# Clustered attention and two MLPs: the second batch's cluster lots spread over the first pair's steps, their loads one by one behind the moves

## The reference

```
q_assign = argmax(q_n . c_n)          k_assign = argmax(k_n . c_n)
mask   = q_assign[..., :, None] == k_assign[..., None, :]
scores = where(mask, scale * q @ k.T, -1e9)
attn   = softmax(scores);  x = attn @ v
x -> x @ w_in (512x2048), h * sigmoid(1.702 h), @ w_out (2048x512)
x -> x @ w_in2 (512x1024), SoLU, layer norm * g_ln, @ w_out2 (1024x512)
```

## Time and profile before

| | |
|---|---|
| median of 3 runs | 667.44 us |
| the profiled execution | 669.38 us, its span 667.5 us (1.88 us around it) |
| PE busy | 640.2 us, 96% of the span |
| DVE, ACT, POOL busy | 465.6, 354.6, 443.1 us |
| granted clock of PE, mean | 0.987 |
| chain that ended last | PE 74%, ACT 10%, issue 6%, DVE 5%, DMA 3% |

### The profile page before, as it was taken

One profiled execution on the slowest core, in us unless ns is written; L12 is line 12 of the kernel. 1 busy time (PEld: TensorE's weight loads), 2 busy tenths in 40 slices (PEclk: granted clock), 3 DMA queues, 4 the chain that ended last, 5 costly groups with the idle time before them and its releaser, 6 DMA issues.

```text
span 667.5 us, 11328 instructions
## 1 busy us (share of the span) xinstructions
PE 640.2 (96%) x3311; PEld 539.5 (81%) x3311; DVE 465.6 (70%) x796; ACT 354.6 (53%) x709; POOL 443.1 (66%) x584
## 2 busy tenths in 40 slices
PE   7779999999999999999999999999999999999998
PEld 4449899898989898888878888878888888888876
DVE  3259999999999996564644684855457478778660
ACT  3149999999999985333325344443332144443241
POOL 3137787987988877766675777676666776867100
PEclk9788999999999999999999999999999999999999
DMA  8946645445545340222222222222220000000001
GB/s 253 281 129 166 148 108 155 123 108 149 135 108 143 91 172 32 95 92 93 99 95 95 90 92 100 96 94 88 100 96 32 0 1 16 33 11 22 32 31 48
DMA packets 26937, 64.32 MB, mean 96 GB/s; under 512 B 3872, under 2 KB 10016, under 8 KB 26912
## 3 DMA queue, kind: packets, MB, share of 16 engines
q1 hardware_dynamic: 25184, 60.87, 31.2%
q10 hardware_dynamic: 1728, 3.15, 1.3%
HBM read 46.51 MB, written 4.72 MB: 77 GB/s over the span
## 4 chain that ended last, share of the span: by engine, by line
PE 74%; ACT 10%; issue 6%; DVE 5%; DMA 3%; DVEq 1%; SPq 1%; POOL 0%; ACTq 0%
PE banks L610 7%; PE banks L640 7%; PE banks L625 7%; PE banks L642 7%; PE banks L627 7%; PE banks L626 7%; PE banks L641 7%; PE banks L595 4%; ACT probs L866 4%; PE banks L770 3%; PE banks L741 3%; PE banks L772 3%; PE banks L739 3%; PE banks L771 3%; PE banks L740 3%
## 5 line engine op out<-in xcount | busy, mean ns | idle before, releaser
L1112 DVE TENSOR_TENSOR probs_tl<-banks,probs_th 128x384 fp32r<-128x384 f32 x192 | 100.6, 547 | 11.8 <-ACT probs_th L877 8.4
L1408 POOL TENSOR_TENSOR wait_scrap<-half_power 128x1 f32<-128x1 f32 x128 | 26.1, 204 | 124.6 <-PE banks L642 67.0
L1092 DVE TENSOR_REDUCE neg_max<-banks 128x1 f32<-128x768 f32 x96 | 91.2, 950 | 7.5 <-PE banks L582 5.5
L877 ACT CAST probs_th<-banks 128x384 fp32r<-128x384 f32 x192 | 83.2, 486 | 21.9 <-PE banks L595 20.4
L866 ACT ACTIVATE probs<-banks,neg_max 128x768 f32<-128x768 f32 x96 | 88.2, 919 | 6.1 <-DVE neg_max L1092 6.0
L1484 POOL TENSOR_SCALAR probs<-probs,row_inv 128x768 f32<-128x768 f32 x96 | 87.0, 907 | 0.0
L1086 DVE TENSOR_TENSOR gl<-gate,gh 128x512 fp32r<-128x512 f32 x48 | 40.3, 839 | 63.5 <-ACT gh L851 63.5
L595 PE MATMUL banks<-ident,probs 128*128 128x128 f32 x576 | 80.1, 275 | 0.7 <-DVE hot_t L1064 0.7
L610 PE MATMUL banks<-probs_th,v_parts 128*128 128x384 f32 x192 | 70.4, 367 | 8.9 <-DVE x_sums L1119 8.9
L1467 POOL TENSOR_TENSOR downl<-gelu_raw,downh 128x512 fp32r<-128x512 f32 x48 | 75.8, 1580 | 4.0
L640 PE MATMUL banks<-gh,downh 128*128 128x512 f32 x192 | 76.0, 396 | 0.4 <-POOL downl L1467 0.2
(11 more groups left out here) (152 smaller groups left out, 1437.6 us busy)
## 6 DMA issues: line engine op xcount, KB each, us to landing
gelu_raw<-w_gelu SPq DMA_DIRECT2D x48, 512.0 KB, 3.3
ln_raw<-w_ln SPq DMA_DIRECT2D x8, 512.0 KB, 4.6
pair_t<-q_t SPq DMA_DIRECT2D x4, 768.0 KB, 7.2
kq_raw<-k_t SPq DMA_DIRECT2D x16, 192.0 KB, 3.5
kq_raw<-q_t SPq DMA_DIRECT2D x16, 192.0 KB, 3.6
pair_t<-k_t SPq DMA_DIRECT2D x4, 768.0 KB, 9.7
q_parts<-k_high SPq DMA_DIRECT2D x16, 192.0 KB, 2.6
q_high<-k_high SPq DMA_DIRECT2D x16, 192.0 KB, 3.0
```

The lines of the kernel that those rows point to most:

```text
L1092: nc.vector.tensor_reduce(out=neg_max[:, col], in_=scores[n % 2], op=ALU.max, axis=mybir.AxisListType.XY, negate=True).then_inc(max_done, 1)
L1112: nc.vector.tensor_tensor(probs_tl[half % 2][at], pt_bank(n, c).rearrange("p (t s) -> p t s", t=CH), probs_th[half % 2][at].bitcast(F32), ...
```

## The change

- Lots 4 to 7 all pass through pair 0's steps, one stage a step: lot e has its sims in step e - 3, its tokens in e - 2, ties in e - 1, first in e. Lot 7's ties are in step 6 and its first in step 7.
- Their sims go to PSUM bank 4, their tokens to bank 5, their ties and first to banks 6 and 7 as before; with this come other waits: sims of lot e > 4 wait until lot e - 1's sims have been copied, tokens of lot e for `compare(e - 1)`.
- The first `turn` (step 6) waits for `compared` = 8 alone, that of step 7 for `ties_t_copied` = 8, and `hot_t_done` = 8 is waited for in step 9.
- `keep_warm` ahead of the first scores is 20 turns in one piece.
- On SP the third move of head 0's k stands ahead of head 1's k and q; the load of lot 5 stands behind head 0's cluster rows, that of lot 6 behind head 1's third move, that of lot 7 behind head 1's last cluster rows, v and gains behind that.

```diff
-        def sims_t_ps(e):
-            return sims[e % 2] if e >= LATE_LOT else banks[:, e % 4, 0:HALF]
+            return banks[:, 4 if e >= 4 else e, 0:HALF]
+        def sims_ps(e):
+            return sims[1 if e >= 4 else e % 2]
-        SIMS_STEP = {6: 1, 7: 3}
...
+        SIMS_STEP = {e: e - 3 for e in range(4, LOTS)}
+        TOKENS_STEP = {e: e - 2 for e in range(4, LOTS)}
+        TIES_STEP = {e: e - 1 for e in range(4, LOTS)}
+        FIRST_STEP = {e: e for e in range(4, LOTS)}
                 move(q_parts[j][high, :], k_low[j][high, :], low_moved[j])
-                if isinstance(it, int) and it == 0 and j == 0:
+                sp.wait_ge(high_moved[j], (it + 1) * 32)
+                move(k_high[j][high, :], k_high[j][low, :], qk_ready[j])
+                if first and j == 0:
                     load_kq(0, 1)
                     load_pairs(4)
-                sp.wait_ge(high_moved[j], (it + 1) * 32)
-                move(k_high[j][high, :], k_high[j][low, :], qk_ready[j])
-                if isinstance(it, int) and it == 0 and j == 0:
-                    load_pairs(5)
+                if first and j == 1:
+                    cluster_rows(q_high[j][D:AUG, :], 0)
+                    load_pairs(6)
                 sp.wait_ge(low_moved[j], (it + 1) * 16)
-                for x, rows in enumerate((q_high[j], k_low[j])):
-                    cluster_rows(rows[D:AUG, :], x)
+                if not (first and j == 1):
+                    cluster_rows(q_high[j][D:AUG, :], 0)
+                cluster_rows(k_low[j][D:AUG, :], 1)
...
             place_head(0, 0)
-            for e in range(6, LOTS):
-                load_pairs(e)
-            sp.dma_start(gains_sb[:], gains).then_inc(gains_loaded, 16)
+            load_pairs(5)
+            place_head(0, 1)
+            load_pairs(7)
             for j in range(2):
                 load_v(0, j)
-            place_head(0, 1)
+            sp.dma_start(gains_sb[:], gains).then_inc(gains_loaded, 16)
...
             first_of(3)
-            sims_of(4)
-            keep_warm(6)
-            tokens_of(4)
-            sims_of(5)
-            ties_of(4)
-            tokens_of(5)
-            first_of(4)
-            keep_warm(16)
+            keep_warm(20)
...
                     if first and n == TURN_LAG + AHEAD:
+                        pe.wait_ge(compared, LOTS)
+                    if first and n == TURN_LAG + AHEAD + 1:
+                        pe.wait_ge(ties_t_copied, LOTS)
+                    if first and n == HEAD_LAG + AHEAD + CH - 1:
                         pe.wait_ge(hot_t_done, LOTS)
```

On ACT, in `attention_turn`:

```diff
+                    if isinstance(it, int) and it == 0 and TURN_LAG < n == TIES_STEP[LOTS - 1]:
+                        copy_ties(LOTS - 1)
                     if exists(it, n, TURN_LAG, STEPS) and not (drain and n >= TURN_LAG):
                         turned_high(*lagged(it, n, TURN_LAG, STEPS))
```

More of the change, by code:

```diff
@@ L88, in clustered_attention_two_mlps @@
         LOTS = 4 * B
-        LATE_LOT = LOTS - 2
         sims_max = [sb(f"sims_max{r}", [P, CH * H], F32, cluster) for r in range(2)]
@@ L384, in place_head @@
                 h = it * 2 + j
+                first = isinstance(it, int) and it == 0
                 low, high = slice(0, D), slice(D, P)
@@ L391, in cluster_rows @@
                     src = mask_heads[x, bass.ds(h, 1)].rearrange("o c s -> (o c) s")
-                    if isinstance(it, int) and it == 0:
+                    if first:
                         sp.wait_ge(hot_t_done, 2 * (x + 1))
@@ L494, in sims_of @@
                 pe.wait_ge(pair_loaded[x][c], (b + 1) * 16)
[L495 to L500, removed]
+                if e == 4:
+                    pe.wait_ge(compared, 3)
+                if e > 4:
+                    pe.wait_ge(sims_t_copied, e)
                 dst = sims_t_ps(e)
@@ L509, in tokens_of @@
                 pe.wait_ge(sims_t_copied, e + 1)
-                if e >= 2:
+                if e >= 4:
+                    pe.wait_ge(compared, e)
+                elif e >= 2:
                     pe.wait_ge(compared, e - 1)
@@ L514, in tokens_of @@
                     t = c * CH + i
-                    last = nc.tensor.transpose(sims[c][:, i * P:(i + 1) * P], sims_t[x][:, t * P:(t + 1) * P],
+                    last = nc.tensor.transpose(sims_ps(e)[:, i * P:(i + 1) * P], sims_t[x][:, t * P:(t + 1) * P],
                                                ident[:])
@@ L683, in attention_turn @@
                             head_half(*lagged(it, n, lag, STEPS), c)
-                    for e in range(5, LOTS):
-                        if first and SIMS_STEP.get(e) == n:
-                            sims_of(e)
+                    for e in range(4, LOTS):
+                        if first and FIRST_STEP[e] == n:
+                            first_of(e)
                         if first and TIES_STEP[e] == n:
                             ties_of(e)
[L689 to L692, removed]
+                        if first and TOKENS_STEP[e] == n:
+                            tokens_of(e)
+                        if first and SIMS_STEP[e] == n:
+                            sims_of(e)
                     if drain and n in UP_STEPS:
@@ L830, in _ @@
             kq_high(0, 1)
-            copy_sims(4)
-            copy_sims(5)
-            copy_ties(4)
             def up_high(at, u):
@@ L904, in attention_turn @@
                         x_high(it - 1, X_STEPS.index(n))
-                    for e in range(5, LOTS):
-                        if isinstance(it, int) and it == 0 and COPY_TIES_STEP[e] == n:
+                    for e in range(4, LOTS):
+                        if isinstance(it, int) and it == 0 and TIES_STEP[e] == n <= TURN_LAG:
                             copy_ties(e)
-                        if isinstance(it, int) and it == 0 and SIMS_STEP.get(e) == n:
+                        if isinstance(it, int) and it == 0 and SIMS_STEP[e] == n:
                             copy_sims(e)
@@ L1049, in compare @@
             def compare(e):
-                sim, r = heads(sims[e % 2]), e % 2
+                sim, r = heads(sims_ps(e)), e % 2
                 dve.wait_ge(sims_done, e + 1)
@@ L1074, in _ @@
             choose(3)
-            compare(4)
-            compare(5)
-            choose(4)
             def gated(at, u):
@@ L1127, in attention_turn @@
                         row_max(it, n)
-                    for e in range(5, LOTS):
-                        if isinstance(it, int) and it == 0 and CHOOSE_STEP[e] == n:
+                    for e in range(4, LOTS):
+                        if isinstance(it, int) and it == 0 and FIRST_STEP[e] == n:
                             choose(e)
-                        if isinstance(it, int) and it == 0 and COMPARE_STEP.get(e) == n:
+                        if isinstance(it, int) and it == 0 and TOKENS_STEP[e] == n:
                             compare(e)
```

6 lines of the change are left out of this document (removed).

## The result

The changed kernel is slower: 675.74 us, the median of 6 runs (673.16 to 677.00), beside 668.88 us for the kernel before on the same chip (6 runs, 667.19 to 670.01). The ratio is 1.0104, with a 95% interval of 1.0079 to 1.0129. A second measurement gave 675.49 beside 668.73, ratio 1.0110 [1.0084, 1.0135]. The forecast was 672.7, with 669.5 to 675.5 as its own range and 666.5 to 677.0 as the range of eight in ten. Both medians lie in the wide range, and the first lies 0.2 above the narrow one.

What follows compares the result with a forecast made beforehand. PE was taken as the bound, busy 96% of the span, so the shift of pair 1's scores counts: +3.3 and clock +2.0 make +5.3 on 667.4, 672.7 us. Own range 669.5 to 675.5; eight in ten 666.5 to 677.

Steps and rivals of the forecast that it cites:

- lot 6's load issued / landed: On SP behind head 1's third move: issued at 30.6, landing at 35.4, from 33.5 to 36.5.
- PE free for it: PE reaches lot 6's sims 7.6 us after pair 0's first scores, at 33.2.
- PE idle in step 3: PE stands 2.2 us for lot 6's load, absorbing everything in front of it.
- from lot 6's landing to lot 7 compared: PE and DVE work on lots 6 and 7: 8.3 us, between 7.0 at full clock and 10.2 at the lower.
- from compare to last choose: Turns, casts, exp, copies and scores stand behind lot 7's compare: 9.7 us, where 2.8 stood before.
- pair 1's scores: Pair 1's first scores on PE come at 65.7 for 62.38, 3.3 us later.
- PE idle there: PE stands about 6 us ahead of pair 1's scores, which without the chain would be due at 59.2.
- The chain: From last choose through mask rows and head 2's moves to pair 1's scores: 12.3 us, hidden before with 1.1 to spare.
- The earlier start: Pair 0's first scores come at 25.6 for 32.45, 6.9 us earlier, absorbed by the wait in step 3.
- The clock term: PE's clock falls to 0.50 behind the wait for pair 1: 2.0 us lost, at most 2.6.
- the rival of the slow clock: Clock stays low from the start or after step 3's idle: last choose 56.1, pair 1 at 68.4, 676.0 us; chance 0.20.
- the loads come in time: Lot 6 has landed by 33.2, so pair 1 comes 0.9 us earlier: 668.5 us, no difference; chance 0.15.

Runs made afterwards that it cites:

- x10: The changed kernel itself, timed and profiled again with no edit: 675.49 us, ratio 1.0110 to the kernel before.
- x1: Changed kernel, with SP placing pair 1 before it waits for the last choose and stores batch 1's mask rows: 669.77 us, ratio 1.0013.
- x3: Changed kernel, with lot 6's first and lot 7's ties and first, their copies and chooses, ahead of the first turn: 665.86 us, ratio 0.9964.
- x5: Kernel before the change, with the same SP edit as x1: 668.38 us, ratio 1.0003.
- x11: Changed kernel with the edits of x1 and x2 together; lot 7's end stays behind the first turn: 665.72 us, ratio 0.9963.
- x12: Changed kernel with the edits of x1, x2 and x3 together: 661.65 us, ratio 0.9897.
- x4: Changed kernel with SP's whole DMA order as in the kernel before, keeping the new order of PE, ACT and DVE: 673.26 us, ratio 1.0074.
- x7: Changed kernel with 36 transposes of the identity on PE in its wait ahead of pair 1's first scores: 672.70 us, ratio 1.0071.
- x2: Changed kernel with the loads of lots 6 and 7 right behind lot 5's, ahead of head 1's moves: 672.01 us, ratio 1.0050.
- x6: Changed kernel with the edits of x3 and x2 together: 663.66 us, ratio 0.9928.
- x9: x6 with 52 instead of 20 keep_warm turns ahead of pair 0's first scores: 664.06 us, ratio 0.9918.

## Why the prediction was right, and where it was not

The way and the mechanism were right. The size fell short: +6.9 us on the same chip where +5.3 was forecast. Of the 3.0 us between 672.7 and 675.74, 1.4 are the kernel before itself, at 668.88 beside the change and 667.44 in the forecast.

| step of the prediction | forecast | first profile | x10's profile |
|---|---|---|---|
| pair 0's first scores | 25.6 | 25.26 | 25.24 |
| lot 6's load issued / landed | 30.6 / 35.4 | 30.60 / 35.80 | 31.93 / 37.2 |
| PE free for it | 33.2 | 34.19 | 33.82 |
| PE idle in step 3 | 2.2 | 1.61 | 3.48 |
| from lot 6's landing to lot 7 compared | 8.3 | 6.9 | 8.3 |
| lot 7 compared | 43.7 | 42.70 | 45.54 |
| from compare to last choose | 9.7 | 9.73 | 9.73 |
| last choose ends | 53.4 | 52.43 | 55.27 |
| from there to pair 1's scores | 12.3 | 12.28 | 12.18 |
| pair 1's scores | 65.7 | 64.71 | 67.45 |
| PE idle there | about 6 | 4.52 | 4.62 |

- **The chain was found and sized right.** What bounds pair 1 is the last choose and 12.3 us behind it; x1 and x3, which attack the two halves of that path, take 6.0 and 9.9 us back, and x5 shows that it was hidden before. That the 9.7 us between compare and choose came out to 0.03 is partly luck. In the chain above, lot 6's first and lot 7's ties, the second turn and the scores take 4.2 us (46.25 to 47.61, 48.14 to 51.00), where the full-clock sum had 2.3. DVE takes 1.0 for the 1.8 put ahead of the choose, since its two turned_low ran beside PE (49.59 to 50.79). The two errors nearly cancel.
- **The late end costs in a second way, which the prediction didn't price.** It followed lot 7's end only into the chain of DMAs. PE's wait for the copy of lot 6's ties and the low clock behind it cost some 4 us more once the chain is gone (x11 and x12). The changed kernel's own time doesn't show this apart, as PE waits 4.52 us for the chain anyway.
- **The steps at the start ran slower than summed.** PE was to be free for lot 6's sims 7.6 us behind pair 0's first scores, by full-clock durations; it took 8.9 (25.26 to 34.19) and 8.6. The granted clock from 20 to 32 was 0.72. So the idle in step 3 was shorter than forecast in the first profile, though the load landed 0.4 later.
- **From there to lot 7's compare, both branches occurred.** The 8.3 stood between 7.0 at full clock and 10.2 at the lower one. The first execution took 6.9, with a clock of 1.00 from 32 to 44; x10's took 8.3, with 0.50 behind the longer wait.
- **The earlier start was absorbed, as forecast.** x4 starts 2.1 us later and is level at the first turn.
- **PE's idle time at pair 1 was too long,** about 6 us (65.7 less 59.2 is 6.5) for 4.52. The prediction let the third turn follow the compare by 7 us; it followed by 8.4 (42.70 to 51.09), because the copy of lot 6's ties (1.92 of waiting) and the low clock behind it lie ahead of it. From the third turn to the last it took 8.3 us (51.09 to 59.37), for the 7.9 of before (53.87 to 61.81). Without the chain pair 1 would have been due near 60, not 59.2.
- **The clock term was mis-sized for the profile, 2.0 for 1.2** (29.18 less 27.98 from pair 1's scores to the mark). Pair 1 itself came at +2.33 for the +3.3 forecast. Together +3.5 where +5.3 stood, within the forecast's own range.
- **The median is further off than the forecast, where the first profile is nearer: +6.9 for +5.3.** The term that was mis-sized there is the landing of lot 6's load, taken as one number. It was taken at 35.4 with a top of 36.5, and in x10's execution it came at 37.2, with the clock at the lower level behind the longer idle. That is the rival of the slow clock in part: it had the last choose at 56.1 and pair 1 at 68.4, and x10 has 55.27 and 67.45. The spreads fit this: the kernels with this wait (the changed one twice, x1, x3, x7) spread over 3.8 to 5.6 us, those with the spread lots and without it (x2, x4, x6, x9, x11, x12) over 1.0 to 3.5. It is a hint and no more, since the kernel before spreads over up to 4.6 us in 17 runs. By its distance to the kernel before (+6.9) the changed kernel lies between the forecast (+5.3) and the rival (+8.6); which share of its executions is of which kind isn't known from two profiles.
- **The rival "the loads come in time" fell short as a rescue.** x2 is that case: 672.0 us, and not the 668.5 that the prediction gave it, as PE then waits for ACT's copy (3.27) instead. The 9.0 us from compare to choose became 11.1: a chain of several engines doesn't move as one.
- By the fit in the Trainium skill (DMA: Bandwidth & Descriptors, Anatomy of one DMA) the load of 768 KB would take 3.8 us, an estimate. That section gives the fit for DMAs that GpSimd issues, and this one is issued by SP, which the prediction doesn't say. The trace has 5.2 from 30.60 to 35.80, and 5.3 in x10; the row of before (4.8) was nearer. PE was free for it at 34.19 (35.80 less 1.61), so by the page it would have stood 0.2 us.

## What to carry to other kernels

When stages are spread over the steps of a pipeline, ask of the last item not when its first stage comes but what hangs on its last. Here the spread of the early stages was a gain (x3, x6). The ends of lots 6 and 7, queued among two turns, an exp and the scores on three engines, took 9.7 us instead of 2.8. They delayed a 12 us chain of DMAs that had 1 us of slack, and made PE wait among the turns. And look at what the consumer really needs: pair 1 used the masks of one batch and waited for both, which cost nothing (x5) until the other end moved (x1). A load issued just in time, behind a wait for other transfers, can cost more than its lateness: in x10 it came 1.5 us later than in the first execution, and pair 1 came 2.7 later.

## What the runs showed of the hardware

- **Identity transposes hold PE's clock.** In x7, 36 of them in 4.09 us kept the granted clock at 1.00 through the wait and behind it; in x9, 52 of them kept it at 1.00 from 20 to 32. The Trainium skill (TensorE: Matmul & The Clock Gate, Part 4: PE-mode transpose) says that such work doesn't count as busy in the same way, which spoke for one rival of the prediction; these rows show no such effect.
- **Equal busy time doesn't mean equal clock.** From 44 to 52 PE was busy 5.51 us in the changed kernel and 5.69 in x3 (24 and 33 matmul records), with a granted clock of 0.57 and 1.00. The changed kernel had PE idle for 1.66 us ahead of that stretch and then for 1.92 within it; in x3 the waits near it were 0.77, 0.55 and 0.57. What decides isn't shown.
- **The same program's DMAs came over 1 us apart in two executions:** head 1's third move, which waits for two moves behind lot 5's load, went out at 29.46 and 30.79.
